# Keys stored without gaps, and each head's keys turned by a matmul of its own

## The chip, the cores and the metric

The kernel runs on one NeuronCore of a Trainium2 chip. The metric is the time of one execution on the device, in microseconds (us). The kernel before took 862.91 us, the median of three runs (859.82 to 865.6).

## The reference

The inputs are q, k and v of 4 batches, 8 heads, 768 tokens and 48 features, and a beta per token. Attention is a delta rule, token by token, with a 48 x 48 state per batch and head (32 of them):

```python
k_n = k / (np.linalg.norm(k, axis=-1, keepdims=True) + 1e-06)
for t in range(S):
    kt, vt, bt = (k_n[:, :, t], v[:, :, t], beta[:, :, t, None])
    y[:, :, t] = np.einsum('bhd,bhde->bhe', q[:, :, t], state)
    v_old = np.einsum('bhde,bhd->bhe', state, kt)
    state = state + bt[:, :, :, None] * np.einsum('bhd,bhe->bhde', kt, vt - v_old)
```

What follows works on the output seen as 4 x 768 x 384: a Fourier transform over tokens and features whose real part is added, a normalization with a two-layer feed-forward block of width 1536, and then a mixing step with sines and cosines of `x @ w_theta`, two 768 x 768 token matrices and a last 384 x 384 layer. All of it is float32 outside.

## The kernel before

**Attention** takes the 768 tokens in 12 chunks of 64. The 32 states are 16 pairs: partitions 0 to 63 (h = 0) hold the chunk's tokens of one half of the heads, partitions 64 to 127 (h = 1) those of the other half. The 16 pairs are again two groups of 8 (r = 0 and 1, `HG` = 8). Within a chunk the recurrence is solved as a triangular system: the products of all keys and queries with all keys (`gram`), an inverse of its 16 x 16 diagonal blocks on VectorE (`blocks_in`, `eliminate`, `scaled_u`, `blocks_out`), three corrections for the blocks above them (`corner`, `solve`, `hop` 1 to 3), the answer (`queried`, `direct`) and the new state (`grow`, read by `predicted` of the next chunk).

**Keys.** `load_k` brings a chunk's keys into `Kb`, six chunks deep, which has for each of 8 pair numbers m and each group r a row of 64 floats: 48 of keys and 16 zeros, that GpSimd wrote once. Two DMAs do it, one per group, in runs of 48 floats. `squares` on GpSimd squares them for the norms, one instruction per group. `grow` uses `key(n, h, r, m)`, a block of 64 tokens by 48 features, as the stationary operand.

**The turn.** `gram`, `queried` and `predicted` need keys with features on the partitions. `turn` makes them: for each m one transpose on TensorE takes 128 tokens by 128 columns, which are the two groups' rows of 48 keys and 16 zeros, and leaves group 0's features at partitions 0 to 47 and group 1's at 64 to 111. Eight of these fill two banks of PSUM, and ScalarE copies each bank to `KQ` (`turned`).

**Order.** Every engine has its instructions written out by hand in one loop over c, from -3 to 11. TensorE's body is: `predicted(c)`, `corner(c)` twice, `solve(c)`, half of `gram(c + 2)`, `hop(c, 1)`, the other half of `gram(c + 2)`, `hop(c, 2)`, `turn(c + 3)`, `hop(c, 3)`, `queried`, `grow`, `direct` twice. Between a hop and the next ScalarE copies its result (`copied_y`) with a mask. In ScalarE's order the masked copies `upper_blocks(c + 2)` stand before `copied_y(c, 2)`, and `turned(c + 3)` between `copied_y(c, 2)` and `copied_y(c, 3)`. Three PSUM banks go round among gram, turn, corner and output products. SyncE issues all loads in a hand-written order, the first keys ahead of the identity that `turn` needs, and ScalarE's queue stores the outputs.

**Dense** (from about 272 us on) is Fourier, feed-forward and mixing, in float16 halves for the large products. Neither its code nor its data are touched by the change.

Of the kernel before, what the change touches and what calls it, by code (L numbers as in the profile page):

```python
# [8 lines left out]
ALU = mybir.AluOpType  # L9
# [3 lines left out]
B, H, S, D = 4, 8, 768, 48  # L13
DM = H * D
FF = 4 * DM
P = 128
# [7 lines left out]
C = 64  # L24
# [59 lines left out]
def attention(nc, A, X, bank, block, sem, ident, preload):  # L84
    with ExitStack() as ph:
        def sb(name, shape, dt=F32):
            return ph.enter_context(nc.sbuf_tensor(name, shape, dt))

        HG = NG // 2
        RK, RT, RA = 6, 4, 3  # L90
        half = (slice(0, C), slice(C, P))
# [5 lines left out]
        KQ = sb("KQ", [P, RT, 2, 2, HG, C])  # L97
        Yo = sb("Yo", [P, 2, NG, D])
        Yv = sb("Yv", [P, 2, NG, D])
        Kb = sb("Kb", [P, RK, HG, 2, C])  # L100
        ET = sb("ET", [P, NG, C])
        TT = sb("TT", [P, NG, C])
        Dy = sb("Dy", [P, BLK, NG, 2])
# [6 lines left out]
        kk = sb("kk", [P, 2, NG, D])  # L110
# [15 lines left out]
        s_zk, s_zs = sem("K_zeros"), sem("S_zeros")  # L126
        s_kd = [sem(f"k_loaded{i}") for i in range(RK)]
        s_vd = [sem(f"v_loaded{i}") for i in range(2)]
        s_qd = [sem(f"q_loaded{i}") for i in range(RT)]
        s_kk, s_n2, s_sq, s_nr = sem("k_squared"), sem("k_norm2"), sem("k_norm"), sem("k_scale_steps")  # L130
# [15 lines left out]
        def there(n):  # L146
            return 0 <= n < NC
# [18 lines left out]
        def grp(a):  # L166
            return slice(a * HG, a * HG + HG)
# [9 lines left out]

        TILES = ((0, 0), (1, 1), (0, 1), (1, 0))

        def keys(n, r):  # L180
            return Kb[:, n % RK, :, r, 0:D]

        def key(n, h, r, m):
            return Kb[half[h], n % RK, m, r, 0:D]

        def moves_of(c):
            if c < NC // 2:
# [6 lines left out]
        def last_store(eng, a):  # L194
            for h in range(2):
                ft = slice(h * (DM // 2), (h + 1) * (DM // 2))
                for row, cnt, tile, p0 in moves_of(LAST):
                    eng.dma_start(X[p0:p0 + cnt, tile, 2 * a:2 * a + 2, ft],
                                  Yo[h * C + row:h * C + row + cnt, LAST % 2, grp(a)].rearrange("p (b g) d -> p b g d", b=2)
                                  ).then_inc(s_ol[a], 16)  # L200
# [5 lines left out]
        @block.sync  # L206
        def _(sp):
            def load_k(n):
                if there(n):
                    if n >= RK:  # L210
                        sp.wait_ge(s_S, n - RK + 1)
                    for r in range(2):
                        sp.dma_start(keys(n, r), A["k"][:, n, grp(r)]).then_inc(s_kd[n % RK], 16)

            def load_v(n):
                if there(n):
                    if n >= 2:
                        sp.wait_ge(s_xe, 2 * (n - 1))
                    sp.dma_start(Vv[:, n % 2], A["v"][:, n]).then_inc(s_vd[n % 2], 16)

            def load_q(n):
                if there(n):
                    if n >= RT:
                        sp.wait_ge(s_O, 2 * (n - RT + 1))
                    for h in range(2):
                        for r in range(2):
                            sp.dma_start(KQ[feat[r], n % RT, 1, h], A["q"][h, :, n, grp(r)]).then_inc(s_qd[n % RT], 16)

            load_k(0)
            sp.dma_start(ident[:], A["ident"]).then_inc(s_id, 16)  # L230
            for src, dst in ((A["beta"], bt[:]), (A["rows"], rows[:])):
                sp.dma_start(dst, src).then_inc(s_cst, 16)
            load_k(1)
            load_q(1)
            load_v(0)
            load_k(2)
            load_v(1)
            load_q(2)
            load_k(3)
            for c in range(C0, NC):  # L240
                load_v(c + 2 if c + 2 > 1 else -1)
                if c >= 0:
                    sp.wait_ge(s_Y, 8 * c + 4)
                load_q(c + 3 if c + 3 > 2 else -1)
                if c >= 0:
                    sp.wait_ge(s_Y, 8 * c + 8)
                load_k(c + 5 if c + 5 > 3 else -1)
                if c == 2:
                    preload(sp)
            sp.wait_ge(s_oe, 2 * LAST + 1)  # L250
            last_store(sp, 0)

        @block.gpsimd
        def _(pool):
            def squares(pair):
                if not 0 <= pair < NC // 2:
                    return
                for n in (2 * pair, 2 * pair + 1):
                    pool.wait_ge(s_kd[n % RK], 32 * (n // RK + 1))
                    if n >= 2:  # L260
                        pool.wait_ge(s_n2, n - 1)
                    for r in range(2):
                        pool.tensor_tensor(kk[:, n % 2, grp(r)], keys(n, r), keys(n, r), ALU.mult).then_inc(s_kk, 1)

            def scaled_v(n):
                if not there(n):
                    return
                pool.wait_ge(s_vd[n % 2], 16 * (n // 2 + 1))
                pool.wait_ge(s_nr, NS * (n // 2) + 5)
                by = ms[:, (n // 2) % 2, (n % 2) * NG:(n % 2 + 1) * NG]  # L270
                pool.tensor_tensor(Vv[:, n % 2], Vv[:, n % 2], by.unsqueeze(2).broadcast_to([P, NG, D]),
                                   ALU.mult).then_inc(s_vp, 1)

            def mask_p(n):
                if not there(n):
                    return
                if n == 0:
                    pool.wait_ge(s_cst, 16 * 5)
                for i, u in enumerate((0, 2, 1, 3)):
                    pool.wait_ge(s_ab, 4 * n + i + 1)  # L280
                    p = PT[:, n % RA, 4 * u:4 * u + 4]
                    mk = mP[:, 0 if n < NC // 2 else 1, :].unsqueeze(1).broadcast_to([P, 4, C])
                    pool.tensor_tensor(p, p, mk, ALU.mult).then_inc(s_pt, 1)  # L283

            pool.memset(Kb[:].rearrange("p n m r d -> p (n m r) d")[:, :, D:C], 0.0).then_inc(s_zk, 1)
            for c in range(C0, NC):
                if c % 2:
                    squares((c + 3) // 2)
                scaled_v(c + 1)
                mask_p(c + 2)  # L290

        @block.tensor
        def _(pe):
# [5 lines left out]
            def take(kind, n, u):  # L299
                at = place[kind, n, u]  # L300
                if at >= 3:
                    pe.wait_ge(*freed(uses[at - 3]))
                return ring(kind, n, u)

            def turn(n):
                if not there(n):
                    return
                pe.wait_ge(s_kd[n % RK], 32 * (n // RK + 1))
                if n == 0:
                    pe.wait_ge(s_zk, 1)  # L310
                    pe.wait_ge(s_id, 16)
                for i in range(2):
                    out = take("T", n, i)[:].rearrange("p (h m t) -> p m h t", h=2, m=HG // 2)
                    for j in range(HG // 2):
                        m = i * HG // 2 + j
                        mm = pe.transpose(out[:, j], Kb[:, n % RK, m].rearrange("p r d -> p (r d)"), ident[:])
                    mm.then_inc(s_T, 1)

            def gram(n, parts):
# [58 lines left out]
            def queried(c):  # L378
                if c < 0:
                    return None  # L380
                out = [take("O", c, a)[:, 0:HG * D].rearrange("p (g d) -> p g d", g=HG) for a in range(2)]
                if c:
                    for m in range(HG):
                        for h, r in TILES:
                            mm = pe.matmul(out[r][half[h], m], KQ[feat[r], c % RT, 1, h, m], Sv[feat[r], c % 2, h * HG + m],
                                           start=m == 0, stop=False, skip_group_check=True)
                    mm.then_inc(s_oq, 1)
                return out
# [26 lines left out]
            for c in range(C0, NC):  # L415
# [10 lines left out]
                out = queried(c)  # L426
# [119 lines left out]
        def _(dve):  # L546
            def norm(pair):
                if not 0 <= pair < NC // 2:
                    return
                if pair:  # L550
                    dve.wait_ge(s_nr, NS * pair)
                for m in range(2):
                    dve.wait_ge(s_kk, 2 * (2 * pair + m + 1))
                    dve.tensor_reduce(nr[:, 0, m * NG:(m + 1) * NG], kk[:, m], AX.X, ALU.add).then_inc(s_n2, 1)

            def scale(pair):
# [1150 lines left out]
```

## Time and profile before

| | us |
|---|---|
| median of three runs | 862.91 |
| the profiled execution, as timed | 864.81 |
| its span in the trace | 862.9 |
| TensorE busy with matmuls | 790.3 |
| TensorE loading weights | 553.4 |
| VectorE busy | 510.7 |
| ScalarE busy | 319.6 |
| GpSimd busy | 162.0 |

Matmuls and weight loads run side by side, so the two TensorE rows are not to be added. A float32 matmul stands in the trace as two MATMUL and two LDWEIGHTS records. The page's slices of time show TensorE busy for 5 to 8 tenths up to about 270 us and for 9 or more in nearly all slices after 300 us. "Issue" in an answer of the trace is time in which the engine waited for nothing that the profile shows.

### The profile page before, as it was taken

To read this page: it belongs to the slowest core of one execution; us is meant where nothing else is said; L and a number is where in the kernel's file an instruction comes from. 1 tells how busy PE (TensorE), PEld (TensorE's weight loads), DVE (VectorE), ACT (ScalarE), POOL (GpSimd) and SP (SyncE) were. 2 spreads that over 40 slices of the span, in tenths; PEclk is the share of its full clock that TensorE was granted. 3 is DMA by queue.
4 is the path that set the end of the run, shared out by engine and by line. 5 is a ranking of instruction groups with operands and counts; after the bars stand their busy time and mean duration, and the time that the engine had idled before them with its cause. 6 is when DMAs were issued, how large, how long until landed. Compare 5 with 4: busy or idle time off the path is not lost.

```text
span 862.9 us, 24837 instructions
## 1 busy us (share of the span) xinstructions
PE 790.3 (92%) x10976; PEld 553.4 (64%) x10976; DVE 510.7 (59%) x1212; ACT 319.6 (37%) x635; POOL 162.0 (19%) x195
## 2 busy tenths in 40 slices
PE   4588788888896999999999999999999999999997
PEld 4588787888885456665666556665656666665664
DVE  5998677777842774643364236455555767758522
ACT  3365455655542252222222223322342444433211
POOL 5242223231200100300030001002121323323100
PEclk9999999999999999999999999999999999999999
DMA  8033533332101232010001001000000000000101
GB/s 202 20 95 77 136 74 83 85 77 58 41 23 54 68 110 83 1 56 1 28 28 47 10 28 28 1 1 2 1 1 1 1 29 19 19 19 28 38 28 47
DMA packets 45048, 37.70 MB, mean 44 GB/s; under 512 B 27401, under 2 KB 39052, under 8 KB 44940
## 3 DMA queue, kind: packets, MB, share of 16 engines
q1 hardware_dynamic: 38020, 30.95, 12.9%
q10 hardware_dynamic: 6920, 5.15, 2.2%
q8 instruction: 87, 1.43, 0.7%
q14 instruction: 21, 0.17, 0.1%
HBM read 26.65 MB, written 4.72 MB: 36 GB/s over the span
## 4 chain that ended last, share of the span: by engine, by line
PE 78%; DVE 11%; issue 5%; ACT 3%; DMA 2%; SPq 1%; POOL 0%; DVEq 0%; ACTq 0%
PE bank L296 13%; PE bank L1018 6%; PE bank L1066 5%; PE bank L1065 5%; PE bank L1019 5%; PE bank L1020 5%; PE bank L1064 5%; PE bank L1002 3%; PE bank L1004 3%; PE bank L1003 3%; PE bank L328 2%; PE bank L952 2%; DVE hT_lo L1436 2%; PE bank L958 2%; PE bank L1042 1%
## 5 line engine op out<-in xcount | busy, mean ns | idle before, releaser
L1184 ACT ACTIVATE hT_hi<-bank 128x384 f16<-128x384 f32 x96 | 46.7, 489 | 161.0 <-PE bank L1004 161.0
L1436 DVE SCALAR_TENSOR_TENSOR hT_lo<-bank,hT_hi 128x384 f16<-128x384 f32 x96 | 53.2, 555 | 73.8 <-ACT hT_hi L1184 73.5
L1018 PE MATMUL bank<-wA,hT_hi 128*128 128x384 f16 x288 | 94.1, 327 | 2.8 <-DVE hT_lo L1436 2.8
L1002 PE MATMUL bank<-unT,wA 128*128 128x384 f16 x288 | 94.1, 327 | 0.4 <-DVE hT_lo L1436 0.4
L1003 PE MATMUL bank<-unT,wA 128*128 128x384 f16 x288 | 94.0, 326 | 0.0
L1019 PE MATMUL bank<-wA,hT_hi 128*128 128x384 f16 x288 | 94.0, 326 | 0.0
L1004 PE MATMUL bank<-unT,wA 128*128 128x384 f16 x288 | 94.0, 326 | 0.0
L1020 PE MATMUL bank<-wA,hT_lo 128*128 128x384 f16 x288 | 94.0, 326 | 0.0
L296 PE MATMUL bank<-Yv,ET 64*64 64x48 f32 x2304 | 75.8, 219 | 6.3 <-issue 3.5
L296 PEld LDWEIGHTS bank<-Yv,ET 64*64 64x64 f32 x2304 | 73.1, 135 | 9.3 <-ACT Yv L434 4.7
L434 ACT ACTIVATE Yv<-bank,rows 128x384 f32<-128x384 f32 x72 | 40.5, 577 | 71.1 <-PE bank L296 70.9
L1444 DVE SCALAR_TENSOR_TENSOR X<-bank,X 128x384 f32<-128x384 f32 x24 | 13.4, 558 | 84.6 <-PE bank L1020 84.6
L283 POOL TENSOR_TENSOR AP<-AP,mP 128x256 f32<-128x256 f32 x48 | 34.3, 736 | 130.2 <-ACT AP L434 130.2
L909 POOL TENSOR_SCALAR fourier_temps<-fourier_temps 128x384 f32<-128x384 f32 x24 | 20.1, 837 | 165.3 <-DVE fourier_temps L1471 165.3
L1066 PE MATMUL bank<-wt_hi,z_first 128*128 128x384 f16 x144 | 47.0, 327 | 0.0
L1065 PE MATMUL bank<-wt_lo,z_first 128*128 128x384 f16 x144 | 47.0, 326 | 0.0
L1066 PE MATMUL bank<-wt_hi,wA 128*128 128x384 f16 x144 | 47.0, 326 | 0.0
L1064 PE MATMUL bank<-wt_hi,wA 128*128 128x384 f16 x144 | 47.0, 326 | 0.0
L1064 PE MATMUL bank<-wt_hi,z_first 128*128 128x384 f16 x144 | 47.0, 326 | 0.0
L1065 PE MATMUL bank<-wt_lo,wA 128*128 128x384 f16 x144 | 47.0, 326 | 0.0
L1018 PEld LDWEIGHTS bank<-wA,hT_hi 128*128 128x128 f16 x288 | 28.1, 98 | 22.5 <-DVE hT_lo L1436 3.4
L1208 ACT ACTIVATE fourier_temps<-fourier_temps,halfpi 128x384 f32<-128x384 f32 x24 | 14.8, 615 | 74.2 <-POOL fourier_temps L909 74.2
(198 smaller groups left out, 1679.7 us busy)
## 6 DMA issues: line engine op xcount, KB each, us to landing
Kb<-k_dram SPq DMA_DIRECT2D x24, 192.0 KB, 3.6
Vv<-v_dram SPq DMA_DIRECT2D x12, 384.0 KB, 3.8
z_first<-w_dram SPq DMA_DIRECT2D x8, 576.0 KB, 4.1
z_first<-wt_dram SPq DMA_DIRECT2D x8, 576.0 KB, 3.7
out_dram<-hT_hi SPq DMA_DIRECT2D x24, 192.0 KB, 1.9
KQ<-q_dram SPq DMA_DIRECT2D x44, 96.0 KB, 2.3
X<-Yo ACTq DMA_DIRECT2D x12, 192.0 KB
X<-Yo ACTq DMA_DIRECT2D x10, 189.0 KB
```

Source lines behind the costliest of these rows:

```text
L296: mm = pe.matmul(out[half[h]], a[half[h]], b[half[h]], start=first, stop=last, skip_group_check=True)
L1002: pe.matmul(out, w1[0][:, k, cols], unT[0][:, k, :], start=(k == 0), stop=False)
L1003: pe.matmul(out, w1[0][:, k, cols], unT[1][:, k, :], start=False, stop=False)
L1004: mm = pe.matmul(out, w1[1][:, k, cols], unT[0][:, k, :], start=False, stop=(k == KD - 1))
L1018: pe.matmul(out, hT[0][:, f, cols], w2[0][:, f, :], start=(f == 0), stop=False)
L1019: pe.matmul(out, hT[0][:, f, cols], w2[1][:, f, :], start=False, stop=False)
L1020: mm = pe.matmul(out, hT[1][:, f, cols], w2[0][:, f, :], start=False, stop=(f == KF - 1))
L1064: pe.matmul(out, zh, wt[0][:, c, t, cols], start=first, stop=False)
L1065: pe.matmul(out, zh, wt[1][:, c, t, cols], start=False, stop=False)
L1066: mm = pe.matmul(out, zl, wt[0][:, c, t, cols], start=False, stop=last)
L1184: act.activation(hT[0][:, f, :], bank[3 + m % 3][:, 0:TG * P], ACT.Relu).then_inc(s_hh, 1)
L1436: dve.scalar_tensor_tensor(hT[1][:, f, :], bank[3 + m % 3][:, 0:TG * P], 0.0, hT[0][:, f, :], ALU.max, ALU.subtract).then_inc(s_hl, 1)
```

## The change

`Kb` now has, for each of six chunks and each group r, one row of 8 x 48 floats with no gaps and 16 floats of zeros at its end. `load_k` is one DMA whose runs are 384 floats. `squares` is one instruction per chunk in place of two, and the semaphores of both are counted accordingly. The memset writes 12 x 16 floats per partition in place of 96 x 16.

With heads side by side, 64 columns that begin at head m hold its 48 keys and the first 16 of the next head (of the zeros, for the last). `turn` makes for each m and each r a float32 matmul: these 128 tokens by 64 columns are the stationary operand, the 128 x 128 identity is the moving one, and the result goes to 64 of the output's partitions, 0 to 63 for r = 0 and 64 to 127 for r = 1. The rows behind the 48 features hold another head's keys instead of zeros, and nobody reads them.

```diff
-        Kb = sb("Kb", [P, RK, HG, 2, C])
+        KW = HG * D + C - D
+        Kb = sb("Kb", [P, RK, 2, KW])
...
-        def keys(n, r):
-            return Kb[:, n % RK, :, r, 0:D]
+        def keys(n):
+            return Kb[:, n % RK, :, 0:HG * D]
 
         def key(n, h, r, m):
-            return Kb[half[h], n % RK, m, r, 0:D]
+            return Kb[half[h], n % RK, r, m * D:(m + 1) * D]
...
-                    for r in range(2):
-                        sp.dma_start(keys(n, r), A["k"][:, n, grp(r)]).then_inc(s_kd[n % RK], 16)
+                    sp.dma_start(keys(n), A["k"][:, n].rearrange("p (r g) d -> p r (g d)", r=2)).then_inc(s_kd[n % RK], 16)
...
-                    for r in range(2):
-                        pool.tensor_tensor(kk[:, n % 2, grp(r)], keys(n, r), keys(n, r), ALU.mult).then_inc(s_kk, 1)
+                    pool.tensor_tensor(kk[:, n % 2].rearrange("p (r g) d -> p r (g d)", r=2), keys(n), keys(n),
+                                       ALU.mult).then_inc(s_kk, 1)
...
-            pool.memset(Kb[:].rearrange("p n m r d -> p (n m r) d")[:, :, D:C], 0.0).then_inc(s_zk, 1)
+            pool.memset(Kb[:, :, :, HG * D:KW], 0.0).then_inc(s_zk, 1)
...
                         m = i * HG // 2 + j
-                        mm = pe.transpose(out[:, j], Kb[:, n % RK, m].rearrange("p r d -> p (r d)"), ident[:])
+                        for r in range(2):
+                            mm = pe.matmul(out[half[r], j], Kb[:, n % RK, r, m * D:m * D + C], ident[:], start=True, stop=True,
+                                           skip_group_check=True)
                     mm.then_inc(s_T, 1)
```

TensorE's program around the turn, of the kernel before. In a name the first tile written is before the arrow, `ET` is the masked corner product, `Yv` the hop's operand.

```order
L328 MATMUL bank<-KQ 64x128 x16
L296 MATMUL bank<-Yv,ET 64x48 x32
L316 MATMUL bank<-ident,Kb 128x2x64 x8
L296 MATMUL bank<-Yv,ET 64x48 x32
L411 MATMUL bank<-Yv,Kb 48x48 x32
```

The same place of the changed kernel (later lines have moved down by two).

```order
L330 MATMUL bank<-KQ 64x128 x16
L296 MATMUL bank<-Yv,ET 64x48 x32
L317 MATMUL bank<-ident,Kb 64x2x64 x16
L296 MATMUL bank<-Yv,ET 64x48 x32
L413 MATMUL bank<-Yv,Kb 48x48 x32
```

The place of the turn is the same, and 16 matmuls stand where 8 transposes were. SyncE's queue begins so before the change:

```order
L213 DMA Kb<-k_dram 128x8x48 x2
L230 DMA ident<-ident_dram 128x128
L232 DMA bt<-beta_dram 128x192
L232 DMA rows<-rows_dram 128x11
L213 DMA Kb<-k_dram 128x8x48 x2
```

and so with it:

```order
L213 DMA Kb<-k_dram 128x2x384
L230 DMA ident<-ident_dram 128x128
L232 DMA bt<-beta_dram 128x192
L232 DMA rows<-rows_dram 128x11
L213 DMA Kb<-k_dram 128x2x384
```

One DMA fewer stands ahead of the identity, and two fewer in all ahead of what follows the second chunk's keys.

## Rows read from the trace of the kernel before

**Rows 1.** The page's chain that ended last, share of the span by engine.

```profile
PE 78%; DVE 11%; issue 5%; ACT 3%; DMA 2%; SPq 1%; POOL 0%; DVEq 0%; ACTq 0%
```

**Rows 2.** Waits of TensorE, 40 to 272 us: total us, times, longest us.

```profile
PE bank L296 <- issue: 16.2, 17, 1.5
PE bank L351 <- issue: 7.2, 6, 2.6
PE bank L328 <- issue: 2.7, 4, 1.1
PE bank L296 <- ACT Yv L434: 2.6, 6, 1.3
PE bank L411 <- issue: 1.6, 2, 1.1
```

**Rows 3.** TensorE busy (records), its loads, VectorE, ScalarE, GpSimd; clock, DMA, GB/s.

```profile
40.00:272.00 232.00, 198.86 (x7271) 191.29 (x7262) 166.28 (x512) 125.64 (x244) 55.75 (x66) 0.99 0.28 72
```

**Rows 4.** Timeline of TensorE from one wait to the next: start, us, what, records.

```profile
178.15 1.36 PE L296 MATMUL bank<-Yv,AP 64*64 64x48 f32 x40 [1.26 <-issue]
...
179.35 1.15 PE L351 MATMUL bank<-Sv,KQ 48*64 48x48 f32 x62
180.29 0.81 PE L296 MATMUL bank<-TT,AP 64*64 64x64 f32 x21
182.13 1.44 PE L296 MATMUL bank<-TT,AP 64*64 64x64 f32 x42 [1.03 <-issue]
```

**Rows 5.** The page's DMA queues: packets, MB, share of 16 engines.

```profile
q8 instruction: 87, 1.43, 0.7%
```

**Rows 6.** The turn's and gram's lines alone: records, ns min/median/max.

```profile
L316 PE MATMUL bank<-ident,Kb x96: 272/273/474, 6.7 to 213.4; 128*128 128x128 f32 x96
L328 PE MATMUL bank<-KQ x768: 266/270/473, 9.3 to 230.5; 48*64 48x128 f32 x192
```

**Rows 7.** Timeline of TensorE: a turn, half a gram, the chunk without a turn.

```profile
130.10 1.06 PE L316 MATMUL bank<-ident,Kb 128*128 128x128 f32 x8 [0.65 <-issue]
131.09 2.01 PE L296 MATMUL bank<-Yv,ET 64*64 64x48 f32 x62
...
188.68 0.33 PE L328 MATMUL bank<-KQ 48*64 48x128 f32 x2
...
189.63 2.22 PE L296 MATMUL bank<-Yv,ET 64*64 64x48 f32 x64
...
233.88 2.36 PE L296 MATMUL bank<-Yv,ET 64*64 64x48 f32 x62 [1.33 <-ACT Yv L434]
```

**Rows 8.** Timeline of the start: what the first block of VectorE waits for.

```profile
6.66 1.94 PE L316 MATMUL bank<-ident,Kb 128*128 128x128 f32 x8 [6.66 <-DMA ident<-ident_dram]
...
9.29 1.99 PE L328 MATMUL bank<-KQ 48*64 48x128 f32 x32 [0.69 <-ACT KQ L434]
...
12.29 1.99 PE L328 MATMUL bank<-KQ 48*64 48x128 f32 x32 [1.01 <-ACT AP L434]
...
14.33 1.09 ACT L434 ACTIVATE AP<-bank 128x512 f32<-128x512 f32 x2 [1.70 <-PE bank L328]
...
15.45 1.36 ACT L434 ACTIVATE Dy<-AP,rows 128x256 f32<-128x256 f32 x2
15.80 0.66 DVE L580 SCALAR_TENSOR_TENSOR cT<-cx,rows,cT 128x32 f32<-128x32 f32 x1
...
16.38 2.22 DVE L594 SCALAR_TENSOR_TENSOR Dy<-AP,rows,Dy 128x256 f32<-128x256 f32 x2
```

**Rows 9.** Stretches with one key load, one value load: busy, clock, DMA share, GB/s.

```profile
121.00:122.00 1.00, 0.53 (x18) 0.53 (x20) 0.83 (x5) 0.00 (x0) 0.00 (x0) 1.00 0.78 303
134.30:136.30 2.00, 2.00 (x99) 2.00 (x89) 1.86 (x5) 1.40 (x4) 0.00 (x0) 1.00 1.00 194
```

**Rows 10.** SyncE's last key load, and a wait of TensorE behind it.

```profile
174.59 1.02 SPq L213 DMA_DIRECT2D Kb<-k_dram  x2
...
197.80 1.78 PE L296 MATMUL bank<-Yv,AP 64*64 64x48 f32 x55 [0.87 <-issue]
```

More of the change, by code:

```diff
@@ L258, in squares @@
                 for n in (2 * pair, 2 * pair + 1):
-                    pool.wait_ge(s_kd[n % RK], 32 * (n // RK + 1))
+                    pool.wait_ge(s_kd[n % RK], 16 * (n // RK + 1))
                     if n >= 2:
                         pool.wait_ge(s_n2, n - 1)
-                    for r in range(2):
-                        pool.tensor_tensor(kk[:, n % 2, grp(r)], keys(n, r), keys(n, r), ALU.mult).then_inc(s_kk, 1)
+                    pool.tensor_tensor(kk[:, n % 2].rearrange("p (r g) d -> p r (g d)", r=2), keys(n), keys(n),
+                                       ALU.mult).then_inc(s_kk, 1)
             def scaled_v(n):
@@ L307, in turn @@
                     return
-                pe.wait_ge(s_kd[n % RK], 32 * (n // RK + 1))
+                pe.wait_ge(s_kd[n % RK], 16 * (n // RK + 1))
                 if n == 0:
@@ L552, in norm @@
                 for m in range(2):
-                    dve.wait_ge(s_kk, 2 * (2 * pair + m + 1))
+                    dve.wait_ge(s_kk, 2 * pair + m + 1)
                     dve.tensor_reduce(nr[:, 0, m * NG:(m + 1) * NG], kk[:, m], AX.X, ALU.add).then_inc(s_n2, 1)
```

## The prediction

> **What bounds the kernel now.** I read the page's chain first: TensorE is 78% of what ended last, VectorE 11%, and 5% is "issue" [rows 1]. The change touches attention alone, so I asked for TensorE's waits from 40 to 272 us, where attention runs in its steady rhythm. There its idle time is nearly all issue: the four lines make 27.7 us in 29 waits, 0.96 us each, against 2.6 us for ScalarE [rows 2]. The reader should see that these waits come at equal distances. Between the one that ends at 178.15 us and the one that ends at 182.13 us stand 40, 62 and 21 matmul records and a few of three short pieces left out between them [rows 4], 126 records, and as many weight loads: 252 instructions, with a few records missing. The page has 87 packets of TensorE's instruction queue for 1.43 MB, 16 KB each [rows 5]; TensorE's 10,976 matmuls and as many loads divided by 87 are 252 too. So I read a wait as the arrival of the next block of about 256 instructions. A stretch of 232 us has 7,271 matmul records [rows 3], 14,542 instructions, 56.8 blocks, hence 0.49 us of waiting per block on the average, and a block whose end is waited for takes 3.98 us [rows 4]. In attention TensorE has therefore two prices: the time of its array and the number of its instructions. What the change adds is priced in both.
>
> **The turn, on the array.** It runs with TensorE's other work in order and nothing beside it. Eight transposes take 0.99 us from start to start of the next hop, 130.10 to 131.09 us [rows 7]. No row shows a matmul of 128 rows by 64 columns. The nearest is gram: 64 columns of weights, 128 moving, float32, on four tiles of the array, and its half of 16 matmuls takes 0.95 us from 188.68 to 189.63 us [rows 7]: four rounds at 0.237 us. Two of gram's four tiles lie in the same rows and differ in columns, as the two groups' tiles now do. So I take a round of two at 0.237 us, 8 rounds, 1.90 us: 0.91 us more per turn. The other end is 16 rounds of one, 3.79 us, 2.80 us more; a lower end is what the transposes take now, nothing more.
>
> Nine turns lie in the steady part. What covers some of it: the next hop needs ScalarE's masked copies. In the first of the three chunks without a turn the hop waits 1.33 us for ScalarE [rows 7]; all six such waits are 2.6 us [rows 2], so behind the nine turns 1.3 us of cover is left. 9 x 0.91 - 1.3 = **6.9 us**. The second PSUM bank of the turn is full only at its end, ScalarE copies it while the next hop's first half runs, and nothing waits for it before the next chunk.
>
> **The turn, in instructions.** A transpose is one matmul record (96 of them, 8 x 12), a float32 matmul two (768 for gram's 384) [rows 6], each with its load. A turn goes from 16 instructions to 64, 48 more, 432 in the nine. That is 1.7 blocks. At the mean wait of 0.49 us per block: **0.8 us**. Bounds: nothing, if the longer turn is time in which the supply catches up, and 1.7 x 3.98 = 6.8 us, if the supply alone sets the pace.
>
> **The start.** Before about 37 us the trace lists full clock, but gram's 32 records take 1.99 us [rows 8] against 0.95 for 32 later, so the array runs as at its lower level of 1.2 GHz, and a round costs 0.498 us. The first turn starts when the identity lands, 6.66 us. One key DMA fewer stands ahead of it; two take 1.02 us to issue [rows 10], so it starts 0.5 us sooner. It takes 8 x 0.498 = 3.98 instead of 1.94 us [rows 8], and gram starts 1.5 us later, at 10.8 us, and ends at 12.8. Its copy by ScalarE is now late by itself (it had waited for the norms' root, which is why the second half came only at 12.29 us, 1.01 us after the first [rows 8]); the second half starts near 13.3 us, 1.0 us later than now, and the two AP copies and the masked Dy copies move by the same. VectorE's first block starts at 16.38 us, held until 16.46 us by cT too [rows 8], and would be ready for Dy some 0.2 us earlier. So it starts **0.8 us** later, and passes this on, since it works almost without a pause until TensorE's first correction. Bounds: 1.3 us if the identity lands no sooner, and 0.5 us gained if the shorter runs bring it 1.3 us sooner still. The turns of chunks 1 and 2 lie in TensorE's idle time there and cost nothing; that cover is far longer than 2 us.
>
> **The key loads, squares and zeros.** A key load of 0.39 MB runs at 194 GB/s with the engines' share at 1.00, where the values' 3 KB runs move 303 GB/s at 0.78 [rows 9]. So a load shrinks from 2.0 to 1.3 us of all engines. In the steady part it is issued a chunk or more ahead of the squares that wait for it, so I cost it at nothing. One square in place of two does the same elements on GpSimd, and the norm needed both anyway; the memset is done before the keys land. Nothing is queued behind a new wait: the change adds none.
>
> **The sum**: 6.9 + 0.8 + 0.8 = 8.5 us. Against the profiled execution, timed 864.81 us, that is 873.3; this execution lies 1.9 us above the median of the runs shown, and on the median the forecast is **871.4 us**, 0.99% slower. Own range: 868 (twice the cover, no price for instructions, start 0) to 874 (no cover, a full wait of 0.96 us per new block, start 1.3).
>
> **Rivals.** (1) *The tiles do not overlap.* For it: each round would then be a single matmul, and two tiles that span all rows occur nowhere in this trace. Against it: gram's four tiles share rows in pairs and still take one round for four. It would cost 9 x 2.80 - 1.3 = 23.9, 0.8 for instructions, and at the start 16 x 0.498 = 8.0 us in place of 3.98, 4.8 in all: 29.5 us, **892.4 us**. The Trainium skill, "TensorE: Matmul & The Clock Gate", Part 3, says that a weight load overlaps matmuls in flight only when their row groups differ; the two tiles of a turn share all row groups, so by that rule the sum would be this rival's or more. Gram's rows [rows 7] speak against the rule where tiles have 64 rows; with 128 rows no row here decides.
>
> (2) *Supply alone sets the pace.* Then new instructions cost whole blocks, 6.8 us, and the array's time is not wholly hidden behind them, since the block with the turn is a slow one anyway: 6.9 + 6.8 + 0.8 = 14.5 us, **877.4 us**. For it: waits end nearly every second block. Against: the other half end without one.
>
> (3) *The key loads hold up the instructions*, the side on which it is not slower. A key load keeps all 16 DMA engines busy for 2.0 us, and the instruction block must pass the same engines. If its short runs are what makes the next block late, each of the seven key loads issued after 40 us gives back up to the 0.96 us of a wait, 6.7 us, and the start gains 2 x 0.7 from two faster loads and keeps its 0.8. That is 8.9 against 8.5 us: **862.5 us**. It decides from 0.9 us per load on. Against it: the last key load is issued at 174.59 us, and the wait that ends at 197.80 us, in a chunk with no key load, is still 0.87 us [rows 10].
>
> **Chances.** Forecast's mechanism 0.58, rival 1 0.12, rival 2 0.18, rival 3 0.12. A measurement of this kernel tells about 1% (8.6 us, above 871.5) from no change. The forecast lies on that line: I give 0.25 of its 0.58 to more than 1% slower, with rivals 1 and 2 that is 0.55, and I shade it to 0.50, because the cover may be longer than the listed waits. Faster by over 1% needs rival 3 and a hidden turn together: 0.06. Within 1%: 0.44. The range takes in rival 3 and rival 2 with the runs' scatter and leaves out rival 1: 862 to 880.
>
> **What would show it.** A turn of 16 matmuls (32 records) near 1.9 us from start to start, and no hop waits for ScalarE behind turns, show the first term; 3.8 us shows rival 1. Issue waits in attention near 28 us in sum and distances still of 256 instructions show the second; 33 us or more would be rival 2, under 22 us rival 3. VectorE's first Dy block near 17.2 us shows the third. The forecast is wrong if the turn costs no more than the transposes, or if the dense part changes.

## The result, and the profile after

The changed kernel takes 865.26 us (median of 20 runs, 861.64 to 869.56), the kernel before 860.43 us in the 20 runs beside them: a ratio of 1.0057, 95% interval 1.0038 to 1.0076. It is slower, by about 4.9 us (3.3 to 6.5), and the forecast of 8.5 us was too much by 3.6 us. The profiled execution was timed 865.82 us with a span of 864.0 us, 1.1 us more than the span shown of before. That earlier execution was one of the longer ones of its kernel (864.81 us against a median of 860.43), so the two traces tell where time went better than how much.

The page of the changed kernel: busy time by engine, the DMA queues, the chain.

```profile
PE 802.4 (93%) x11264; PEld 565.0 (65%) x11264; DVE 512.3 (59%) x1212; ACT 320.7 (37%) x635; POOL 160.0 (19%) x183
...
DMA packets 23355, 37.73 MB, mean 44 GB/s; under 512 B 2634, under 2 KB 17357, under 8 KB 23245
...
q8 instruction: 89, 1.46, 0.7%
...
PE 81%; DVE 10%; issue 4%; ACT 2%; DMA 2%; ACTq 0%; SPq 0%; DVEq 0%
```

TensorE has 288 matmul records more (12 turns of 24) and is busy 12.1 us longer. There are about half as many DMA packets (23,355 where before had 45,048) for nearly the same bytes, and two more instruction packets. The chain has more of TensorE and less issue than [rows 1].

The turn of chunk 7 in the changed kernel's timeline, and the first chunk without a turn.

```profile
130.14 1.97 PE L317 MATMUL bank<-ident,Kb 128*64 128x128 f32 x32
132.04 1.14 PE L296 MATMUL bank<-Yv,ET 64*64 64x48 f32 x32
...
233.25 2.01 PE L296 MATMUL bank<-Yv,ET 64*64 64x48 f32 x62 [1.24 <-ACT Yv L436]
```

From 130.14 to 132.04 us are 1.90 us for 16 matmuls: the eight rounds of 0.237 us that gram's rows [rows 7] gave. Two tiles of 128 rows and 64 columns do work side by side, and rival 1 is out. The rule weighed there (the Trainium skill, "TensorE: Matmul & The Clock Gate", Part 3: a load overlaps matmuls only where row groups differ) does not hold in this trace: the two tiles share every row group, and in the 1.90 us lie 32 LDWEIGHTS records with a median of 137 ns, 4.4 us if they stood in a row, beside 32 MATMUL records of 273 ns.

TensorE's waits, 40 to 272 us, after the change; then its row of busy time for that stretch.

```profile
PE bank L296 <- issue: 11.2, 16, 2.0
PE bank L353 <- issue: 5.5, 6, 1.8
PE bank L413 <- issue: 2.8, 4, 1.1
PE bank L296 <- ACT Yv L436: 1.2, 1, 1.2
PE bank L330 <- issue: 1.2, 1, 1.2
```

```profile
40.00:272.00 232.00, 207.62 (x7562) 200.92 (x7558) 170.87 (x519) 128.08 (x246) 55.13 (x58) 0.99 0.25 74
```

The issue waits of four lines sum to 20.7 us where before they made 27.7 [rows 2], although there are more instructions: 7,562 matmul records, 59.1 blocks, 0.35 us of waiting per block instead of 0.49. They are still waits for blocks: between any two issue waits of more than 0.5 us in this stretch, TensorE's matmul and load records count a whole multiple of about 253, in the trace of before (25 such waits) as in this one (17). ScalarE's waits behind turns are gone, as forecast. In 232 us TensorE is 8.8 us busier than in [rows 3].

Where attention ends and the dense part begins:

```profile
279.03 4.19 PE L954 MATMUL bank<-fourier_tables,fourier_temps 128*128 128x385 f32 x6 [7.23 <-DVE fourier_temps L1328]
```

In the trace of before this group starts at 279.78 us (its line is shown with the next experiment). So in this pair of traces attention ends 0.75 us sooner with the change, and what makes the span longer is the dense part, 585.0 us instead of 583.1, which the change does not touch. The next experiment shows where that comes from. The 4.9 us rest on the 20 runs of each kernel, not on these two traces.

The start after the change, to be read against [rows 8].

```profile
1.25 0.45 SPq L230 DMA_DIRECT2D ident<-ident_dram  x1
...
6.00 3.68 PE L317 MATMUL bank<-ident,Kb 128*64 128x128 f32 x32 [6.00 <-DMA ident<-ident_dram]
...
10.40 1.08 ACT L436 ACTIVATE KQ<-bank 128x512 f32<-128x512 f32 x2 [4.76 <-DMA mE<-mE_dram]
...
11.54 1.98 PE L330 MATMUL bank<-KQ 48*64 48x128 f32 x32 [1.85 <-ACT KQ L436]
...
14.33 1.99 PE L330 MATMUL bank<-KQ 48*64 48x128 f32 x32 [0.81 <-ACT AP L436]
...
18.27 2.34 DVE L596 SCALAR_TENSOR_TENSOR Dy<-AP,rows,Dy 128x256 f32<-128x256 f32 x2 [2.21 <-ACT Dy L436]
```

The identity lands 0.66 us sooner (0.5 forecast). But ScalarE copies nothing before 10.40 us: its order has a wait for all mask tables ahead of the loop, and the last of them, `mE`, came at 7.94 us before. It holds ScalarE 0.7 us beyond the end of the first turn. The second key load is now issued at 2.69 instead of 3.83 us; that it delays the tables by this is my reading. VectorE's first Dy block starts 1.9 us later than before.

### The profile page after: what moved, and what is told of

It is laid out like the page before. It is cut to its first block, busy times and chain, and to the rows that moved or that the text cites. A ratio compares the mean times of both kernels' runs of the same rounds, so it can differ in the third digit from the quotient of the medians.

```text
span 864.0 us, 25389 instructions
## 1 busy us (share of the span) xinstructions
PE 802.4 (93%) x11264; PEld 565.0 (65%) x11264; DVE 512.3 (59%) x1212; ACT 320.7 (37%) x635; POOL 160.0 (19%) x183
## 2 busy tenths in 40 slices
DMA packets 23355, 37.73 MB, mean 44 GB/s; under 512 B 2634, under 2 KB 17357, under 8 KB 23245
## 4 chain that ended last, share of the span: by engine, by line
PE 81%; DVE 10%; issue 4%; ACT 2%; DMA 2%; ACTq 0%; SPq 0%; DVEq 0%
PE bank L296 14%; PE bank L1020 6%; PE bank L1068 5%; PE bank L1067 5%; PE bank L1022 5%; PE bank L1021 5%; PE bank L1066 5%; PE bank L1004 3%; PE bank L1006 3%; PE bank L1005 3%; PE bank L330 2%; PE bank L954 2%; DVE hT_lo L1438 2%; PE bank L960 2%; PE bank L317 2%
## 5 line engine op out<-in xcount | busy, mean ns | idle before, releaser
L1004 PEld LDWEIGHTS bank<-unT,wA 128*128 128x128 f16 x288 | 28.1, 98 | 21.7 <-issue 2.5
```

The source lines that it names most:

```text
L1004: pe.matmul(out, w1[0][:, k, cols], unT[0][:, k, :], start=(k == 0), stop=False)
```

## The experiments

Every kernel was timed in five rounds beside the kernel before, in four groups, each on one chip: the kernel before again, the new turn alone (first time), the loads alone and the plain matmuls; then the two split turns, the change again (first time) and the steady turns twice; then the short runs, the change and the new turn alone (both a second time); last the transposes twice. A ratio is to the kernel before in the same group, with its 95% interval.

The expectations weigh theories by letter. **A** is the forecast's way: each added microsecond and each added block are paid (for the loads alone: short runs hold things up). **B** changes its meaning: for the new turn alone and in steady chunks only, it says that the longer turn is paid out of the waits for instructions, which is later called **E**; for the loads, that they are hidden; for the doubled turn, that the supply sets the pace. **C** and **D**: the key loads' short runs do or do not delay the blocks. Four expectations (the short runs, the transposes twice, and the second ones of the new turn alone and of the change) name sums of waits of 26 to 36 us; the four issue lines that are added up below give 20.7 to 29.0 us in all traces, so those figures count something wider, and only differences can be compared.

### The kernel before, again

No edit.

> The kernel before, once more, for a second trace. Both theories: no difference from the kernel before (0.995 to 1.005). If the first trace was typical, the issue waits of TensorE from 40 to 272 us sum to 26 to 30 us again and the wait-to-wait distance is 3.9 to 4.0 us; if it was a slow one (it was timed 864.8 against a median of 860.4), they sum to 22 to 25 us.

0.9992 (0.9969 to 1.0015). The same lines of TensorE's waits, 40 to 272 us:

```profile
PE bank L296 <- issue: 14.7, 16, 1.9
PE bank L351 <- issue: 8.0, 6, 2.8
PE bank L296 <- ACT Yv L434: 2.7, 6, 1.3
PE bank L328 <- issue: 2.5, 2, 1.3
PE bank L411 <- issue: 1.4, 2, 1.1
```

26.6 us of issue: the first trace was typical in this. But the dense part, from the first matmul after the gap to the end, took 585.5 us in this trace against 583.1 in the first trace of the same kernel. The two rows below are that first matmul group, of this run and of the first trace of before.

```profile
279.94 4.19 PE L952 MATMUL bank<-fourier_tables,fourier_temps 128*128 128x385 f32 x6 [6.29 <-DVE fourier_temps L1326]
```

```profile
279.78 3.84 PE L952 MATMUL bank<-fourier_tables,fourier_temps 128*128 128x385 f32 x6 [7.18 <-DVE fourier_temps L1326]
```

The granted clock fell to its lower level in the wait ahead of both, and stayed there for 13.7 us here and 6.8 us there. Over all traces the dense part is 581.9 to 583.1 us after 6.8 us (583.0 after 10.2) and 584.8 to 585.5 us after 13.7 us, with either turn: up to 3 us of a single trace that say nothing of the change. The first trace of the changed kernel had the 13.7 us.

### The new turn alone, on the old layout (twice)

```diff
-                        mm = pe.transpose(out[:, j], Kb[:, n % RK, m].rearrange("p r d -> p (r d)"), ident[:])
+                        for r in range(2):
+                            mm = pe.matmul(out[half[r], j], Kb[:, n % RK, m, r, :], ident[:], start=True, stop=True,
+                                           skip_group_check=True)
```

> The new turn alone, on the old layout with its short-run loads. Theory A, the forecast's sum (turn 6.9, instructions 0.8, start 1.3 without the earlier identity) with a gain from the loads that I had priced at nothing: 9 us slower than before, and 4 us slower than the change. Theory B, the longer turn is time in which the instruction supply catches up and the loads do nothing: as the change, 4 to 5 us slower than before, issue waits down by 6 to 8 us against before.

> The new turn on the old layout and loads a second time (the first was 0.38% slower than before, its part in the nine steady turns alone 0.77%, which cannot both be right). Theory C: as the change with short runs, waits of 33 us or more, 0.9 to 1.2% slower than before. Theory D: as the change, 0.4 to 0.7%.

1.0038 (1.0012 to 1.0063) and 1.0044 (1.0011 to 1.0077): 3 to 4 us slower, where A said 9; the upper ends are 5.5 and 6.6 us. Theory B's number fits the time, but its waits were to fall by 6 to 8 us and fell by 2 at most, to 25.9 and 26.2 us. So most of the loss is the turn's, and by the middle values it is less than half of what its array time and instructions were priced at.

### The loads alone: long runs, old transposes

```diff
-                    for r in range(2):
-                        sp.dma_start(keys(n, r), A["k"][:, n, grp(r)]).then_inc(s_kd[n % RK], 16)
+                    sp.dma_start(Kb[:, n % RK], A["k"][:, n]).then_inc(s_kd[n % RK], 16)
...
-        "k": pairs(inputs["k"], D),
+        "k": np.pad(pairs(inputs["k"], D).reshape(P, NC, 2, NG // 2, D).transpose(0, 1, 3, 2, 4),
+                    ((0, 0),) * 4 + ((0, C - D),)),
```

> The loads alone: the old layout and transposes, but keys arrive from memory with their 16 zeros, one DMA of 4 KB runs per chunk, no memset. Theory A, short runs hold up the start and the instruction blocks: 3 to 4 us faster than before (0.996). Theory B, the loads are hidden: within 1 us of before, the first turn 0.5 to 1 us sooner at the start and nothing else.

1.0066 (1.0040 to 1.0093), slower, which neither theory had. VectorE's first Dy block came at 19.4 us instead of 16.4, and the first steady turn at 48.3 instead of 44.8: 3.5 us of the 5.7 are lost at the start. Two things differ there, a third more bytes (the zeros) while the engines are full, and a second key load that is issued earlier, as in the change; `mE` lands at 11.54 us. The kernel does not tell them apart. No gain by long runs showed anywhere.

### Plain matmuls of 128 columns in place of the transposes

```diff
-                        mm = pe.transpose(out[:, j], Kb[:, n % RK, m].rearrange("p r d -> p (r d)"), ident[:])
+                        mm = pe.matmul(out[:, j], Kb[:, n % RK, m].rearrange("p r d -> p (r d)"), ident[:], start=True, stop=True,
+                                       skip_group_check=True)
```

> The old layout, and plain float32 matmuls of 128 columns in place of the transposes: 8 per turn, 32 instructions (transposes 16, the new turn 64), with the array time of a plain float32 matmul, 8 x about 0.23 us as in the new turn. If array time decides: the same as the new turn on the old layout, within 1.5 us. If the number of instructions decides: a third of that kernel's loss (16 extra instructions of 48).

1.0075 (1.0048 to 1.0102). Its turn's records:

```profile
L316 PEld LDWEIGHTS bank<-ident,Kb x192: 186/192/333, 6.3 to 218.4; 128*128 128x128 f32 x192
L316 PE MATMUL bank<-ident,Kb x192: 274/275/580, 6.3 to 218.5; 128*128 128x128 f32 x192
```

From the turn's first record to the next hop's the nine steady turns sum to 17.8 us, against 17.1 with two tiles and 11.1 with transposes. With half the new turn's instructions it is no faster, rather slower by 0.4% (the intervals overlap). The number of instructions does not decide. Its loss, 6.5 us (4.2 to 8.8), is the whole of the 6.7 us of added turn.

### The new turn in the steady chunks only, and in the first three only (old layout)

```diff
+                        if n < 3:
+                            mm = pe.transpose(out[:, j], Kb[:, n % RK, m].rearrange("p r d -> p (r d)"), ident[:])
+                            continue
                         for r in range(2):
```

and the same with `if n >= 3:`.

> Old layout and loads; the new turn in the nine steady turns (chunks 3 to 11) only, transposes in the first three. Forecast's steady part: 6.9 + 0.8, at most 7.7 us slower than before. Theory B, the longer turn is paid out of the waits for instructions: 0 to 2 us, because the 3.3 us that the new turn cost in all were mostly the start.

> Old layout and loads; the new turn in chunks 0 to 2 only. By the forecast's working of the start, without the earlier identity: 1.3 us slower than before, and VectorE's first Dy block 1.3 us later than its 16.4 us. Theory B: 2 us slower, as the traces of the change (first Dy block 1.9 us later) show, and this is most of the change's loss.

1.0077 (1.0048 to 1.0107) and 0.9998 (0.9969 to 1.0027). The loss lies in the nine steady turns, and theory B's share-out, 0 to 2 us for them, is wrong. The first number, 6.7 us (4.2 to 9.3), would bear out A's 7.7 us, but the kernel with the new turn everywhere on this layout was 0.38% and 0.44% slower; the intervals overlap only from 1.0048 to 1.0063 and to 1.0077. The second says that on this layout, where the tables land as before, the start costs between -2.7 and 2.3 us. Its trace shows why a trace gives no fixed price for the start:

```profile
6.58 3.50 PE L320 MATMUL bank<-ident,Kb 128*64 128x128 f32 x32 [6.58 <-DMA ident<-ident_dram]
10.78 1.10 PE L333 MATMUL bank<-KQ 48*64 48x128 f32 x32 [0.69 <-ACT KQ L439]
```

The half gram behind the longer turn takes 1.10 us instead of the 1.99 us of [rows 8]: here the clock had risen from its lower to its upper level by the end of the first turn. VectorE's first Dy block was back at 16.36 us.

### The change, again (twice)

No edit.

> The changed kernel once more, on the chip of the others. Both theories: 0.4 to 0.8% slower than before. For its trace: if the waits for instructions really shrink with the change, they sum to 19 to 23 us again from 40 to 272 us; if the first trace was a lucky one, to 26 to 30.

> The change a third time, beside the one with short runs. Both theories: 0.6% (0.4 to 0.8) slower than before. Theory C: waits of 26 to 30 us in the steady stretch once more. Theory D: any value up to 35 us.

1.0062 (1.0036 to 1.0087) and 1.0067 (1.0038 to 1.0096). Waits of 23.8 and 23.9 us on issue lines, less than the 27.7 and 26.6 of before; these are the third's.

```profile
PE bank L296 <- issue: 12.9, 15, 1.4
PE bank L353 <- issue: 7.9, 7, 2.8
PE bank L413 <- issue: 2.2, 3, 1.0
...
PE bank L330 <- issue: 0.9, 1, 0.9
```

`mE` landed at 9.91 and 10.07 us, so the late tables belong to the change; VectorE's first Dy block started at 17.8 and 17.1 us. From the first steady turn to the dense part these two took 238.8 and 238.6 us, the first trace of the same kernel 232.2.

### The steady turns issued twice

```diff
-                        for r in range(2):
+                        for r in (0, 1, 0, 1) if n >= 3 else (0, 1):
```

> The change with every matmul of the nine steady turns issued twice into the same place (outputs unchanged): 1.9 us and 64 instructions more per turn than the change. Forecast's way, array time on the path plus half a us per block: 9 x 1.9 + 1.1 = 18 us slower than the change. Theory B, the supply sets the pace and hides array time: 9 x 64 / 256 = 2.25 blocks of 3.9 us, 9 us slower than the change, issue waits down by another 8 us or more.

1.0247 (1.0218 to 1.0276), 16 us above the change in the same group (0.0185 of 865; 12.6 to 19.4 by the two intervals), between the two but far nearer to A's 18 than to B's 9. One of its turns:

```profile
140.62 3.71 PE L317 MATMUL bank<-ident,Kb 128*64 128x128 f32 x64
144.26 1.95 PE L296 MATMUL bank<-Yv,ET 64*64 64x48 f32 x60
```

The second 16 matmuls add 1.74 us to the first 1.90: a round takes 0.218 us, and 0.16 us of a turn are its two edges. From first record to the next hop the nine turns sum to 33.2 us, 16.1 more than the change's: now about every microsecond is paid. Its waits:

```profile
PE bank L296 <- issue: 13.3, 14, 1.8
PE bank L353 <- issue: 8.1, 5, 3.4
PE bank L330 <- issue: 1.4, 3, 0.9
...
PE bank L413 <- issue: 0.3, 1, 0.3
```

23.1 us of issue in a stretch of the same length, 20.7 to 23.9 in the change: nothing more is won back. That the supply sets the pace is out.

### The change with its keys in short runs

```diff
-                    sp.dma_start(keys(n), A["k"][:, n].rearrange("p (r g) d -> p r (g d)", r=2)).then_inc(s_kd[n % RK], 16)
+                    for r in range(2):
+                        sp.dma_start(keys(n)[:, r].rearrange("p (g d) -> p g d", g=HG),
+                                     A["k"][:, n, grp(r), 0:D]).then_inc(s_kd[n % RK], 16)
...
-        "k": pairs(inputs["k"], D),
+        "k": np.pad(pairs(inputs["k"], D), ((0, 0),) * 3 + ((0, C - D),)),
```

> The change, but its keys arrive as before: two DMAs per chunk, in runs of 48 floats (the source has gaps now, the storage none). In the traces so far the waits for instruction blocks in the steady stretch sum to 34 to 36 us where keys arrive in short runs and to 26 to 30 us where they arrive in runs of 384 floats. Theory C, the short runs delay the blocks: waits of 33 us or more, 4 to 6 us slower than the change. Theory D, the difference was the lot of single traces: waits of 28 to 35 us, within 2 us of the change.

1.0049 (1.0025 to 1.0074), beside 1.0067 for the change in the same group, and its waits are

```profile
PE bank L298 <- issue: 11.6, 15, 1.6
PE bank L355 <- issue: 7.8, 7, 2.1
PE bank L415 <- issue: 1.4, 3, 0.6
...
PE bank L332 <- issue: 1.2, 1, 1.2
```

22.0 us, no more than in the change, and no 4 to 6 us slower: C falls. `mE` landed at 8.60 us here, 1.3 to 1.8 us sooner than in the change, whose keys come by one DMA in long runs. Some 21,700 packets more or fewer in a run make no difference here that the intervals show.

### The old transposes issued twice

```diff
-                        mm = pe.transpose(out[:, j], Kb[:, n % RK, m].rearrange("p r d -> p (r d)"), ident[:])
+                        for _ in range(2 if n >= 3 else 1):
+                            mm = pe.transpose(out[:, j], Kb[:, n % RK, m].rearrange("p r d -> p (r d)"), ident[:])
```

> The kernel before, with the transposes of the nine steady turns issued twice into the same place (outputs unchanged): 1.0 us more array time per turn, as the new turn has, but 16 instructions more, not 48, and no tiles. Forecast's way: 9 x 0.99 - 2.2 of cover = 6.7 us, and 0.3 for instructions: 7.0 us slower than before. Theory E, time added in the turn is partly won back from the waits for instruction blocks, whatever form it has: 3 to 5 us slower, waits in the steady stretch down by 1.5 us or more from the 35 us of the kernel before.

1.0027 (0.9999 to 1.0054): 2.3 us (0 to 4.7), not clear of nothing, where A has 7.0. A turn and the waits:

```profile
130.44 1.97 PE L317 MATMUL bank<-ident,Kb 128*128 128x128 f32 x16
132.33 2.01 PE L296 MATMUL bank<-Yv,ET 64*64 64x48 f32 x62
```

```profile
PE bank L296 <- issue: 17.1, 20, 2.4
PE bank L352 <- issue: 5.7, 6, 1.2
PE bank L412 <- issue: 2.8, 3, 1.5
...
PE bank L329 <- issue: 0.2, 1, 0.2
```

The turn takes 1.89 us, as the new one does; the nine sum to 17.1 us, 5.9 more than before, with neither tiles nor many instructions. It costs less than that, and the waits are 25.8 us, 1.9 less than in [rows 2]. The measured time rules A's 7.0 us out and is, if anything, below E's 3 to 5. The waits are down by E's 1.5 us against the first trace of before and by 0.8 against the second (26.6), so how much of the rest came from them rests on single traces.

## Why the forecast was right in kind and too large

The way and the main cause were right: slower, by the array time of nine longer turns. The size was not. The measured 865.26 us lie in the wide range of 862 to 880 us and below the forecast's own range of 868 to 874; the kernel is 0.6% slower, where the largest chance (0.50) stood on more than 1%.

Three places of each trace, in us, and the sum of the four issue lines from 40 to 272 us:

| kernel | first steady turn starts | from there to the dense part's first matmul | issue waits |
|---|---|---|---|
| transposes in the steady turns (before, twice; new turn in the first three only) | 44.8, 44.3, 44.4 | 235.0, 235.6, 235.1 | 27.7, 26.6, 28.3 |
| the loads alone | 48.3 | 236.5 | 29.0 |
| transposes twice | 45.1 | 235.8 | 25.8 |
| new turn, old layout (twice; steady only) | 46.2, 45.0, 45.5 | 240.8, 239.7, 239.4 | 25.9, 26.2, 27.5 |
| plain matmuls | 44.2 | 241.2 | 26.7 |
| the change (three) | 46.8, 46.1, 45.4 | 232.2, 238.8, 238.6 | 20.7, 23.8, 23.9 |
| the change with short runs | 45.2 | 233.2 | 22.0 |
| steady turns twice | 47.9 | 255.0 | 23.1 |

**The turn on the array: right in its rate, a little high in its sum.** 1.90 us per turn was forecast and measured. That it came out to the hundredth has luck in it: by the doubled turn a round takes 0.218 us and the edges 0.16, and in gram's four rounds (0.95 us) the edges are 0.08, just half of that. From first record to the next hop the nine turns grew from 11.1 to 17.1 us in all three traces of the change: 6.0 us, not 6.9. The cover was taken from the idle time listed before the hop (1.3 us), which begins where the modelled end of the last matmul lies; counted from start to start it was 8.2 - 6.0 = 2.2 us.

**The turn in instructions: this step failed.** I priced 48 more instructions at the mean wait of a block and added them to the array's time, 0.8 us on top, and so took the waits of before as fixed. Four traces with transposes in the steady chunks have 26.6 to 29.0 us of issue waits on their four lines. The change has 20.7, 23.8 and 23.9, the new turn on the old layout 25.9, 26.2 and 27.5. They fall where I had them rise, clearly in the change, and on the old layout by little. The twofold transposes show it in time: 5.9 us more of array time cost 2.3 us (0 to 4.7). What was missing, as I read it, is that a longer turn lengthens the time in which the next block can arrive, so the two prices are not to be added. The doubled turn shows the limit: its 16 further us cost 16.

How much is won back is open. The reading that the first 6 us in the turn are paid in part out of waiting that would have come anyway is supported by the twofold transposes, and by the change itself, whose two larger terms make 7.6 us as measured (6.0 and the 1.6 us below) against 4.9 (3.3 to 6.5). It is not supported by two others: the new turn in the steady chunks only cost 6.7 us (4.2 to 9.3) and the plain matmuls 6.5 (4.2 to 8.8), each about the whole of their added array time. The traces cannot settle it. Three executions of the changed kernel differ by 6.6 us from the first steady turn to the dense part, more than the whole effect; some 3 us of that are issue waits, and the clock granted from 40 to 272 us was 0.99, 0.97 and 0.98 in them, so part of it may be the clock's. That a slow stretch lets the supply gain on TensorE is argued, since no trace shows when a block was asked for.

**The start: the right chain, priced low.** Dy was forecast at 17.2 us and came at 18.3, 17.8 and 17.1. The chain was the forecast's, with one wait that I missed: the mask tables on ScalarE's queue land 2.0 to 2.5 us later and hold ScalarE 0.4 to 0.7 us beyond the first turn. The first steady turn starts at 46.1 us in the mean of the three instead of 44.5 in the three traces of the first row: 1.6 us, where 0.8 were forecast, with 1.4 us between executions of the changed kernel.

**The key loads: rightly at nothing** in the steady part (short and long runs differ by 0.2%, the intervals overlap), so rival 3 falls, though the waits below 22 us in the first trace were the sign I had named for it. The sign was wrong, not only the rival: those waits came down with short runs too. Its sum also gave back the start's 0.8 us, which its words keep; with the start's 0.8 us kept it is 863.3 us, not 862.5. Rival 2 would have had 33 us of waits, and falls with them.

**Sum.** 6.0 for the turn and 1.6 for the start are 7.6 us. Less the 3.6 us that the twofold transposes did not cost (5.9 - 2.3; 1.2 to 5.9 by its interval) that makes 4.0 us (1.7 to 6.4), measured 4.9 (3.3 to 6.5). The sum agrees but is no test, since its last term is that wide. Open remains why the waits are lowest where keys are stored without gaps (20.7 to 23.9 us in five traces, against 25.8 to 29.0 in nine on the old layout) while the time on the two layouts is the same within its interval. Keys without gaps with the old transposes would separate them; that was not tried. No version was measurably faster than the kernel before.

## What to carry to other kernels

Where an engine waits for its own instructions at equal distances, do not simply add the price of new instructions to the price of their array time: measure the one with the other held still, by issuing an existing group twice. Take an effect of a few microseconds from medians and not from a pair of traces, which here differed by more in executions of one kernel. Count cover from start to start, not from the idle time that a modelled end leaves. And a change in one queue's loads can make those of the other queue land later, as `mE` did here: list what each engine waits for before its loop.

## What the hardware showed beside

Two tiles of 128 rows by 64 columns run side by side at float32: a turn of eight rounds takes 1.90 us, 0.237 us a round with its edges, the same as for four tiles of 64 by 64 [rows 7], and 0.218 us for each further round. Plain matmuls of 128 columns take 17.8 us for nine turns where the pairs of tiles take 17.1. Float32 transposes of 128 by 128 take about half: eight 0.99 us with the edges [rows 7], eight more 0.90 us.

After the 7 us wait between attention and the dense part the clock stays at its lower level for 6.8, 10.2 or 13.7 us in executions of the same program or of programs alike in that part, worth up to 3 us. In the first 37 us it rose early in some executions and not in others: half a gram behind the first turn takes 1.10 us in one trace and 1.99 us in another.
